# Two score tiles of pair p+2 issued ahead of the value products of pair p in a fused attention and expert kernel

## The reference

```python
scores = scale * np.matmul(q, k.transpose(0, 1, 3, 2))
keep = is_sink | in_window
scores = np.where(keep, scores, -1000000000.0)
a = np.exp(scores - np.max(scores, axis=-1, keepdims=True))
a = a / (np.sum(a, axis=-1, keepdims=True) + 1e-09)
attn = np.matmul(a, v)                       # 2 x 8 x 768 x 64
# then, on x = attn laid out as 1536 x 512:
out += P[:, e:e + 1] * (np.maximum(x @ w1[e], 0.0) @ w2[e])   # for e in 0..7
return (out @ w_a) * (out @ w_b) @ w_out
```

## Time and profile before

| | us |
|---|---|
| median of 3 runs (lowest to highest) | 1502.53 (1501.46 to 1502.85) |
| the profiled execution, its own time | 1502.23 |
| its span, first to last instruction | 1500.4 |
| PE busy in the span | 1461.6 (97%) |
| DVE busy | 596.3 (40%) |
| ACT busy | 330.3 (22%) |
| attention, from the first score matmul to the last turn | about 14.6 to 126.6 |

### The profile page before, as it was taken

One profiled execution on the slowest core, in us unless ns is written; L12 is line 12 of the kernel. 1 busy time (PEld: TensorE's weight loads), 2 busy tenths in 40 slices (PEclk: granted clock), 3 DMA queues, 4 the chain that ended last, 5 costly groups with the idle time before them and its releaser, 6 DMA issues.

```text
span 1500.4 us, 17348 instructions
## 1 busy us (share of the span) xinstructions
PE 1461.6 (97%) x6804; PEld 1189.4 (79%) x6804; DVE 596.3 (40%) x1145; ACT 330.3 (22%) x683; POOL 47.5 (3%) x84
## 2 busy tenths in 40 slices
PE   4889999999999999999999999999999999999999
PEld 3657888888888888888888888888888888888887
DVE  6886444523233332323333232333323334343433
ACT  5775111202021120202112020211202122112211
POOL 4330000000000000000000000000000000000000
PEclk9999999999999999999999999999999999999999
DMA  5211101001010101101010110101011011011002
GB/s 163 96 54 58 57 0 57 34 23 56 0 56 0 56 12 44 56 0 56 0 56 0 56 56 0 56 0 56 1 42 43 0 42 43 0 43 43 0 0 84
DMA packets 41262, 56.28 MB, mean 38 GB/s; under 512 B 2176, under 2 KB 20736, under 8 KB 41216
## 3 DMA queue, kind: packets, MB, share of 16 engines
q1 hardware_dynamic: 36320, 53.26, 10.2%
q10 hardware_dynamic: 4896, 2.41, 0.5%
HBM read 52.51 MB, written 3.15 MB: 37 GB/s over the span
## 4 chain that ended last, share of the span: by engine, by line
PE 92%; ACT 3%; DVE 3%; issue 1%; DMA 1%; POOL 0%; POOLq 0%; SPq 0%; ACTq 0%
PE ps L488 30%; PE ps L490 30%; PE ps L489 30%; ACT pr L731 2%; DVE pr L958 1%; DMA rq<-in_q_dram 1%; PE ps L433 1%; ACT pt L740 0%; DVE pt L967 0%; DVE xl L976 0%; PE ps L511 0%; PE ps L567 0%; DVE wh L921 0%; DVE wl L918 0%; DVE wh L918 0%
## 5 line engine op out<-in xcount | busy, mean ns | idle before, releaser
L488 PE MATMUL ps<-xh,wh 128*128 128x512 f32 x1056 | 411.5, 390 | 0.0
L490 PE MATMUL ps<-xl,wh 128*128 128x512 f32 x1056 | 411.3, 389 | 0.0
L489 PE MATMUL ps<-xh,wl 128*128 128x512 f32 x1056 | 410.8, 389 | 0.0
L488 PE MATMUL ps<-wh,hh 128*128 128x512 f32 x912 | 360.3, 395 | 0.0
L489 PE MATMUL ps<-wh,hl 128*128 128x512 f32 x912 | 359.8, 394 | 0.0
L490 PE MATMUL ps<-wl,hh 128*128 128x512 f32 x912 | 359.8, 394 | 0.0
L712 ACT ACTIVATE hh<-ps 128x512 fp32r<-128x512 f32 x192 | 114.9, 598 | 856.8 <-PE ps L490 855.9
L1152 DVE SCALAR_TENSOR_TENSOR hl<-ps,hh 128x512 fp32r<-128x512 f32 x192 | 132.4, 691 | 347.5 <-ACT hh L712 347.4
L1169 DVE SCALAR_TENSOR_TENSOR acc<-ps,g_now,acc 128x512 f32<-128x512 f32 x168 | 126.1, 751 | 296.4 <-PE ps L490 296.4
L488 PEld LDWEIGHTS ps<-xh,wh 128*128 128x128 f32 x1056 | 198.2, 188 | 42.0 <-issue 0.6
L490 PEld LDWEIGHTS ps<-xl,wh 128*128 128x128 f32 x1056 | 198.2, 188 | 41.6
(11 more groups left out here) (92 smaller groups left out, 550.9 us busy)
## 6 DMA issues: line engine op xcount, KB each, us to landing
raw<-in_w_dram SPq DMA_DIRECT2D x32, 1024.0 KB, 7.0
rk<-in_k_dram SPq DMA_DIRECT2D x8, 384.0 KB, 4.4
rq<-in_q_dram SPq DMA_DIRECT2D x8, 384.0 KB, 5.2
raw<-in_w_a_dram SPq DMA_DIRECT2D x6, 512.0 KB, 3.7
raw<-in_w_b_dram SPq DMA_DIRECT2D x6, 512.0 KB, 4.8
raw<-in_w_out_dram SPq DMA_DIRECT2D x6, 512.0 KB, 5.6
out_dram<-acc SPq DMA_DIRECT2D x12, 256.0 KB, 2.0
vs<-in_v_dram ACTq DMA_DIRECT2D x6, 384.0 KB, 3.3
```

What stands on the lines that cost most here:

```text
L488: nc.tensor.matmul(o, ah, bh, start=first, stop=False)
L489: nc.tensor.matmul(o, al, bh, start=False, stop=False)
L490: return nc.tensor.matmul(o, ah, bl, start=False, stop=last)
```

## The change

In an iteration with 0 <= p <= 5 (six of them), PE's 12 matmuls of score tiles 0 and 1 of pair p+2 come ahead of the value products of pair p. They stood between turn 0 and turn 1 of pair p+1. The programs of DVE, ACT, POOL and SP are the same as before, and so are all semaphores and waits: a moved instruction takes its wait with it.

```diff
                         if p + 1 >= 0:
                             turn(p + 1, q)
-                        if p >= 0 and p + 2 < PAIRS and q < 3:
+                        if p >= 0 and p + 2 < PAIRS and 0 < q < 3:
                             scores(p + 2, (2 * q, 2 * q + 1))
 
                 scores(0, range(QT))
                 for p in range(-1, PAIRS - 1):
                     if p >= 0:
+                        if p + 2 < PAIRS:
+                            scores(p + 2, (0, 1))
                         weigh(p)
                     pair(p)
```

## The result

The changed kernel takes 1532.57 us (median of 4 runs, 1532.23 to 1533.33) against 1502.69 us before (with a fourth run added to the three of the table): a ratio of 1.0201, 95% interval 1.0183 to 1.0218. The direction was as forecast; the size, 30 us instead of 21, lies 3.6 us beyond the upper end of the range. The profiled execution took 1532.23 us, its span is 1530.4 us, so 30.0 us above the span of before.

What follows compares the result with a forecast made beforehand. Attention was taken as bound by a chain through ACT and DVE, PE costing time only where it delivers late. 1502.5 us plus 16.9 for the wait plus 4 for clock falls gave 1523.5 us, range 1517.5 to 1529.

Steps and rivals of the forecast that it cites:

- The wait: On PE, between turn 3 and the moved score tiles: 4.15 us idle in one piece until DVE's split is done.
- The new path of 6.11 us: From the split's end to DVE's first mask, through score tiles, value products, turn 0 and its copy: 6.11 us, before 3.29.
- the difference of 2.82 us an iteration: Growth of the path from the split's end to the first mask; over six iterations 16.9 us.
- the sum: 1502.5 us before plus 16.9 us gives 1519.4; with four more falls of PE's clock 1523.4 us.
- Case B: Rival in attention: PE's wait costs time but brings at most two clock falls, 1518.4 to 1520.5 us; chance 0.20.
- Idle stretch brings falls: PE's idle piece ahead of the moved tiles halves its clock in about five of six iterations, four more than before: +4 us.
- A fall costs 1.0 us: Price of one drop of PE's clock to half rate, from the one slow iteration of before: 14.56 us instead of 13.55.
- at most half of 3.21 us: Upper bound for one clock fall, with the whole slow stretch of PE on the chain: 1.6 us.
- case A: PE's wait plus three to six clock falls of 1.0 to 1.6 us each: 1521.4 to 1528 us; chance 0.60.
- Turn 1 half a turn later, taken as 0: On PE, turn 1 and score tiles 2 and 3 come about 0.5 us later; taken as hidden, otherwise 0.5 us an iteration.
- Case E: Faster: the split is done 2.82 us earlier, so score tiles fill PE's small wait; at most 2 us, 1500.5 us; chance 0.02.

Runs made afterwards that it cites:

- the kernel with fillers: The changed kernel with 16 filler matmuls, result unused, in PE's wait ahead of the moved score tiles, six times: 1520.52 us, ratio 1.0124.
- The early split: Split of pair p+3 made earlier on ACT and DVE, sink columns first on POOL: 1517.20 us on the changed kernel, 1505.54 us on the kernel before.
- the kernel with the tiles behind the products: The kernel before with score tiles of pair p+2 issued behind pair p's value products and ahead of turn 0 of pair p+1: 1502.16 us, ratio 0.9996.

## Why the prediction was right in its mechanism and wrong in its size

- **The wait.** PE 4.15 us idle ahead of the moved tiles was forecast; 4.20 us is there in five iterations, released by the line named, and 2.92 us in the first. That one costs 2.81 us at full clock all the same (turn 3 to turn 3 in 16.68 us against 12.27, of which 1.60 are slow clock).
- **The new path of 6.11 us and the difference of 2.82 us an iteration.** Measured with the clock held: 2.81 us. Times six it is 16.9 us, as in the sum. Case B, the wait without falls, is the kernel with fillers: forecast 1518.4 to 1520.5, measured 1520.5, at the upper edge for the two reasons given there.
- **Idle stretch brings falls.** Right, and more so than I took it: six of six instead of five. The Trainium skill, "TensorE: Matmul & The Clock Gate", Part 1, by which an idle engine falls back to half rate, would have given six, and the trace agrees with it there: six stretches at a granted clock of 0.50.
- **"A fall costs 1.0 us": this is the step that failed.** From the tiles' start to turn 0 the six iterations take 5.90, 7.25, 6.15, 7.27, 6.16 and 7.28 us where full clock takes 4.30: 14.2 us in all, 2.4 us a fall, and 1.6 us was my upper end. With it the sum closes: 16.9 + 14.2 - 1.0 (the fall of before, gone) = 30.1 us, against 30.0 measured between the spans. The price of 1.0 us came from one fall of 3.21 us, two thirds of its possible cost. In the changed kernel five of the six slow stretches last 6.8 us. A stretch costs about half of what PE is busy in it, as all of that work is on the chain: where 6.20 us are busy, 2.95 us are lost (pair 1), and where 3.95 us are, since most of PE's wait falls into the stretch, 1.85 us (pair 2). My bound, "at most half of 3.21 us", took the length of that one stretch for a constant; it is the length that was off, not the half.
- **Range.** Its upper end was case A with six falls at 1.6 us; six at 2.4 us put the time beyond it. I should have read one fall as one sample.
- **Turn 1 half a turn later, taken as 0.** Right: iterations with the clock held show 2.81 us and no more, and so does the kernel with the tiles behind the products.
- **Case E, faster, decided by a split 2.82 us earlier.** The early split did not reach it, since it made PE wait 2.0 us for turn 3; so this break-even was not tried cleanly.

Still open is what decides whether the clock falls and how long it stays low. With the early split PE had an idle piece of 2.0 us an iteration in both kernels, and the clock fell in two of six iterations in one and in all six in the other.

## What to carry to other kernels

A matmul moved up in a hand-written order takes its wait with it: before moving it, compare the end of its operand's producer with the start of everything that it is moved past. Here the operand was ready 0.5 us ahead of the old place and 4.2 us behind the new one. When such a wait opens an idle piece right ahead of critical matmuls, take half clock over their whole length as the upper end of the price, not a fall seen where there was slack. Here that end is 4.3 us an iteration from the tiles to turn 0, and 1.6 to 3.0 were lost. And early work gains only as far as the engines behind it take it early and the next work is early too: the version that did gain 5 us moved tiles, masks and outputs together, and none past the split.

## What the runs showed of the hardware

- A slow stretch can last 6.8 us while PE's records are almost unbroken: 6.20 of 6.82 us busy at a granted clock of 0.50, from 56.40 us on in the changed kernel. Before, it had lasted 3.4 us with PE busy throughout.
- A fall can come within the idle piece: from 73.47 us on in the changed kernel, 1.35 us after PE went idle and 2.86 us before its next matmul.
- An idle piece of 2.0 us ahead of turn 3 brought a fall in two of six iterations with the early split alone, and in six of six with the moved tiles as well.
- At the low level the first run of value products takes 2.40 us instead of 1.30 and the score tiles 1.69 instead of 0.98.
- Filling 2.1 of the 4.2 us ahead of the tiles saved nothing that is clear of the spread (1531.1 us), filling 3.9 us saved all of the clock's share (1520.5 us).
